# Two chained feed-forward layers after a short convolution: 64-row contraction terms as alternating half-array matmuls

## The chip, the cores and the metric

One core of one Trainium2 chip. The metric is the time of one execution on the device in microseconds; the kernel before takes 1338.2 us (median of 3 runs, 1337.74 to 1338.87).

## What is computed

`x` is 2 x 4096 rows of 192; `weight_gen` gives each row 8 heads with 7 taps. Cut to what matters:

```python
w = softmax(weight_gen)                                # over the 7 taps
x1 = einsum('bshk,bskhg->bshg', w, x_unf)              # causal 7-tap convolution, per head
h = np.maximum(x1 @ w_in, 0.0)                         # 192 -> 2048
x2 = h * h @ w_out                                     # 2048 -> 192
h = x2 @ w_in2
out = (h * np.cos(h)) @ w_out2
```

All in float32. On TensorE the kernel keeps the precision by splitting each operand into a rounded part (`_hi`) and the rest (`_lo`) and adding the products hi x hi, hi x lo and lo x hi.

## The kernel before

The 8192 tokens are 16 tiles of 512 (`TOK`). A layer's 2048 inner columns are 16 chunks of 128 (`SLOTS`), so each layer has 256 steps. Step n of layer 1 makes `h1` (one PSUM bank of two) from x1 (`up`, L363 to L370), squares its relu into `g1_hi` and `g1_lo`, and adds it into `y1` two slots later (`down`, L372 to L381). Layer 2 does the same with `h2`, `g2_*` and `y2`, 19 steps behind (`LAG`, L34), since its input x2 is the finished y1 of the tile. The program is a sequence of slots, written out per engine in a fixed order (`slot`, L399, L503, L648): slot i of tile t has step n = 16 t + i of layer 1 and m = n - 19 of layer 2. On TensorE a slot is up 1, down 1, up 2, down 2. The loop runs tiles 2 to 13; tiles 0 and 1 are written out because weights are still loaded and split, and the last four for the tail.

A row has 192 inputs: `DA` = 128 and `DD` = 64. An up is three matmuls over the 128 (L366 to L368), and two for the 64. For these `wd` holds the rounded weights in partitions 0 to 63 and their rest in 64 to 127, and the 64 inputs stand in both halves, so that L369 and L370 are full 128-row matmuls. To fill both halves the weights are loaded twice (L245, L246), x1's last 64 columns are written twice (L328, L643, turned by `turn_x1`), and x2's last 64 are copied to SBUF as `x2_d` and split for both halves (L532, L533 on ScalarE, L688 twice on VectorE), in slot `Y1_AT` + 1. Every matmul has 512 moving columns and its own 128 x 128 weights. A down is five: three into bank 0 of y for output columns 0 to 127, and two into bank 1, whose halves hold two partial sums of the last 64.

What orders the work is a semaphore per result. up 1 of step n waits for `g1_ready` of step n - 2 (its bank is then free), down 1 for `g1_ready` of its own step (L421), up 2 and down 2 likewise with `g2_ready` (L431, L447). up 2 of a new tile (slot `C2` = 3) waits for `x2_split` (L433). After y2 of a tile is done, slot `Y2_AT` = 5 copies it (L516, L661), and slots 6 and 7 transpose it on TensorE through a bank of h2 (`turn_out`, L396), which waits for the g2_lo of the step that used the bank (L441). Slots `TURN` = 13 and 14 transpose the next x1 (L386).

ScalarE and VectorE go through a slot in this order. ScalarE: sin of step m-1 (L510), y2 copy, relu (L521), x2 parts, x1_hi, g2_hi of m-1 (L542), g1_hi (L547), turns (rounding to whole turns, L552), output. VectorE: product with the cosine for m-1 (L655), y2 copy, relu square (L664), x2 and x1 parts, g2_lo of m-1 (L678), g1_lo (L683), x2's last 64 (L688), fraction of a turn (L693), output (L699). GpSimd convolves the next tile (L319, L325) and splits layer 2's weights.

Of the kernel before, what the change touches and what calls it, by code (L numbers as in the profile page):

```python
# [7 lines left out]
def conv_ffn_ffn_kernel(nc, x_d, gen_d, w_in1_d, w_out1_d, w_in2_d, w_out2_d, out_d):  # L8
# [29 lines left out]
    Y2_AT = C2 + D2  # L38
# [10 lines left out]
    INV_2PI = 1.0 / (2.0 * math.pi)  # L49
    assert DD * 2 == P and LAG % 2 == 1 and Y1_AT < C2  # L50
# [23 lines left out]
    with ctx:  # L74
# [12 lines left out]
        wd = [sb(f"wd{l}", [P, FF], F32R) for l in range(2)]  # L87
# [16 lines left out]
        x1 = sb("x1", [P, JJ, 2 * P])  # L104
# [3 lines left out]
        x1_hi = sb("x1_hi", [P, 2, 2, TOK], F32R)  # L108
        x1_lo = sb("x1_lo", [P, 2, 2, TOK], F32R)
        x2_hi = sb("x2_hi", [P, 2, 2, TOK], F32R)  # L110
        x2_lo = sb("x2_lo", [P, 2, 2, TOK], F32R)
# [10 lines left out]
        x2_d = sb("x2_d", [DD, TOK])[:, :]  # L122
# [12 lines left out]
        halo_zeroed = sem("halo_zeroed")  # L135
        ident_ready = sem("ident_ready")
# [39 lines left out]
        x2_d_ready = sem("x2_d_ready")  # L176
# [36 lines left out]

        def piece_lo(eng, pc, op):
# [4 lines left out]
            fs = slice(q * PF, (q + 1) * PF)  # L219
            eng.wait_ge(piece_hi[pc], op + 1)  # L220
            if op:
                eng.wait_ge(piece_ready[pc], op)
            if op == 0:
                last = eng.tensor_tensor(wa_lo[l][:, cols], stage_a[:, r, :], wa_hi[l][:, cols], ALU.subtract)
            elif op == 1:
                last = eng.tensor_tensor(wd[l][DD:P, cols], stage_d[DD:P, r, :], wd[l][DD:P, cols],
                                         ALU.subtract)
# [9 lines left out]
        def _(sp):  # L237
            def load_piece(pc):
# [6 lines left out]
                sp.dma_start(stage_d[0:DD, r, :], w_in_d[l][DA:DM, cols]).then_inc(piece_loaded[r], 16)  # L245
                sp.dma_start(stage_d[DD:P, r, :], w_in_d[l][DA:DM, cols]).then_inc(piece_loaded[r], 16)  # L246
# [30 lines left out]
            sp.wait_ge(first_sum, TAPS)  # L277
# [20 lines left out]
        def _(pool):  # L298
# [5 lines left out]
            STEP = 2 * TAPS - 1  # L304

            def convolve(t):
# [3 lines left out]
                products = [tap[:, k, :].rearrange("p (j d) -> p j d", d=DM) for k in range(2)]  # L310
                total = x1[:, :, 0:DM]
# [3 lines left out]
                for k in range(TAPS):  # L315
# [8 lines left out]
                    if k < TAPS - 1:  # L324
                        pool.tensor_tensor(total, products[0] if k == 1 else total, products[k % 2],  # L325
                                           ALU.add).then_inc(pool_step, 1)

                pool.tensor_tensor(x1[:, :, DM:2 * P], x1[:, :, DA:DM], products[(TAPS - 1) % 2][:, :, DA:DM],  # L328
                                   ALU.add).then_inc(pool_step, 1)
                pool.wait_ge(pool_step, STEP * (t - 1) + STEP)  # L330
                pool.tensor_tensor(total, total, products[(TAPS - 1) % 2], ALU.add).then_inc(x1_ready, 1)
# [30 lines left out]
        def _(pe):  # L362
            def up(o, l, f, hi, lo, par):  # L363

                f = slice(f * P, (f + 1) * P)
                pe.matmul(o, wa_hi[l][:, f], hi[:, par, 0, :], start=True, stop=False)  # L366
                pe.matmul(o, wa_hi[l][:, f], lo[:, par, 0, :], start=False, stop=False)  # L367
                pe.matmul(o, wa_lo[l][:, f], hi[:, par, 0, :], start=False, stop=False)  # L368
                pe.matmul(o, wd[l][:, f], hi[:, par, 1, :], start=False, stop=False)  # L369
                return pe.matmul(o, wd[l][:, f], lo[:, par, 1, :], start=False, stop=True)  # L370

            def down(y, l, f, hi, lo):  # L372
# [3 lines left out]
                part_a, part_d = y[:, 0, :], y[:, 1, :]  # L376
                pe.matmul(part_a, w[:, f, 0:DA], hi, start=first, stop=False)  # L377
                pe.matmul(part_a, w[:, f, 0:DA], lo, start=False, stop=False)  # L378
                pe.matmul(part_a, w[:, f, 2 * P:2 * DM], hi, start=False, stop=final)  # L379
                pe.matmul(part_d, w[:, f, DA:2 * P], hi, start=first, stop=False)  # L380
                return pe.matmul(part_d, w[:, f, DA:2 * P], lo, start=False, stop=final)  # L381

            def turn_x1(bank, part):

                for jj in range(JJ):
                    last = pe.transpose(h1[:, bank, jj * P:(jj + 1) * P], x1[:, jj, part * P:(part + 1) * P],  # L386
                                        ident[:, :])
# [11 lines left out]
            def slot(t, i, par):  # L399
                n = SLOTS * t + i  # L400
                m = n - LAG
                of = 1 - par if i >= C2 else par

                if live(n):
# [8 lines left out]
                    up(h1[:, i % 2, :], 0, i, x1_hi, x1_lo, par).then_inc(up1_done, 1)  # L413

                if TURN <= i < TURN + 2 and tile_live(t + 1) and live(n):
                    pe.wait_ge(x1_ready, t + 1)
                    pe.wait_ge(g1_ready, n)
                    turn_x1((i + 1) % 2, i - TURN).then_inc(x1_turned, 1)

                if live(n - D1):  # L420
                    pe.wait_ge(g1_ready, n - D1 + 1)  # L421
                    if i == D1 and counted(t):
                        pe.wait_ge(y1_read, t)
                    if isinstance(n, int) and n - D1 < SLOTS and (n - D1) % PF == 0:
                        pe.wait_ge(piece_ready[(n - D1) // PF], 3)
                    down(y1, 0, (i - D1) % SLOTS, g1_hi[:, (i - D1) % 2, :],
                         g1_lo[:, (i - D1) % 2, :]).then_inc(down1_done, 1)

                if live(m):
# [8 lines left out]
                    up(h2[:, (i - C2) % 2, :], 1, (i - C2) % SLOTS, x2_hi, x2_lo, of).then_inc(up2_done, 1)  # L438

                if OUT_AT <= i < OUT_AT + 2 and tile_live(t - 2):  # L440
# [19 lines left out]
            pe.wait_ge(first_sum, TAPS)  # L460
# [17 lines left out]
        def _(act):  # L478
            def piece_his(pc):
# [4 lines left out]
                act.wait_ge(piece_loaded[r], 64 * (pc // RING + 1))  # L484
                if l == 1:
                    act.activation(stage_a[:, r, :], stage_a[:, r, :], ACT.Copy,
                                   scale=INV_2PI).then_inc(piece_scaled, 1)
                    act.activation(stage_d[:, r, :], stage_d[:, r, :], ACT.Copy,
# [5 lines left out]
                act.activation(wd[l][:, cols], stage_d[:, r, :], ACT.Copy).then_inc(piece_hi[pc], 1)  # L494
# [8 lines left out]
            def slot(t, i, par):  # L503
# [4 lines left out]
                if live(m - 1):  # L508
                    act.wait_ge(fraction_ready, m)
                    act.activation(wave[:, 1 - c, :], wave[:, 1 - c, :], ACT.Sin,  # L510
                                   scale=2.0 * math.pi).then_inc(cos_ready, 1)
                if i == Y2_AT and tile_live(t - 2):
# [252 lines left out]
```

## Time and profile before

| | before |
|---|---|
| median of 3 runs | 1338.2 us |
| the profiled execution | 1338.88 us |
| its span, first to last instruction | 1337.1 us |
| mean granted TensorE clock | 0.987 |
| TensorE matmuls | 1257.4 us busy, 94% |
| VectorE | 991.4 us, 74% |
| ScalarE | 841.3 us, 63% |
| GpSimd | 379.1 us, 28% |

The profile is of one execution. Times are from the span's start; a line number is that of the kernel before. PE is TensorE's matmuls, PEld its weight loads, DVE VectorE, ACT ScalarE, POOL GpSimd. A recorded matmul is longer than the distance to the next one, since matmuls are pipelined and their ends are modelled: the distance of two starts is what counts. "Idle before" is the time an engine stood still before an instruction, and the releaser is what it had waited for.

### The profile page before, as it was taken

What the parts mean: (1) busy time and instruction counts of PE and PEld (TensorE: products, weight loads), DVE (VectorE), ACT (ScalarE), POOL (GpSimd) and SP (SyncE); (2) the same over time, 40 slices, a digit from 0 to 9 for tenths busy, and PEclk for the clock granted to TensorE, in tenths of its full rate; (3) what the DMA queues carried; (4) which work ended last, traced back from release to release, by engine and by line L of the source; (5) the groups of instructions that cost most, each with busy time, mean ns of one, the idle gap of its engine ahead of it and who ended that gap; (6) DMA issues with size and microseconds to landing.
All of it is one profiled execution on the core that took longest, in us unless ns stands there. A gap on an engine that the chain in (4) does not pass through costs nothing.

```text
span 1337.1 us, 17547 instructions
## 1 busy us (share of the span) xinstructions
PE 1257.4 (94%) x5392; PEld 993.1 (74%) x5392; DVE 991.4 (74%) x1487; ACT 841.3 (63%) x1535; POOL 379.1 (28%) x259
## 2 busy tenths in 40 slices
PE   3779999999999999999999999999999999999986
PEld 2557878778787877878787787878778787877754
DVE  7977777777777777777777777777777777777764
ACT  2487666666666666666666666666666666666654
POOL 3748530606023060502406051240605124000000
PEclk9889999999999999999999999999999999999998
DMA  5230000000100000010000001000000100000000
GB/s 163 79 122 1 30 30 13 30 13 0 41 0 29 12 30 12 0 41 0 30 12 29 12 0 41 0 29 12 30 12 0 41 0 1 13 1 13 1 12 12
DMA packets 14459, 31.80 MB, mean 24 GB/s; under 512 B 1605, under 2 KB 10051, under 8 KB 14273
## 3 DMA queue, kind: packets, MB, share of 16 engines
q1 hardware_dynamic: 14400, 31.19, 7.1%
q14 instruction: 43, 0.34, 0.1%
q8 instruction: 16, 0.26, 0.1%
HBM read 24.89 MB, written 6.29 MB: 23 GB/s over the span
## 4 chain that ended last, share of the span: by engine, by line
PE 60%; DVE 22%; ACT 10%; issue 6%; DMA 1%; ACTq 0%; DVEq 0%; SPq 0%
PE y L380 6%; PE y L378 6%; PE y L377 6%; PE y L381 6%; PE y L379 6%; PE h L366 6%; PE h L368 6%; PE h L370 6%; PE h L369 6%; PE h L367 6%; DVE turns L693 4%; DVE g_lo L678 4%; ACT turns L510 4%; ACT g_hi L542 3%; DVE h L655 3%
## 5 line engine op out<-in xcount | busy, mean ns | idle before, releaser
L319 POOL TENSOR_TENSOR tap<-xc,gen 128x768 f32<-128x768 f32 x105 | 162.0, 1549 | 689.0 <-PE h L386 666.3
L510 ACT ACTIVATE turns<-turns 128x512 f32<-128x512 f32 x256 | 161.9, 632 | 239.1 <-DVE turns L693 228.8
L655 DVE TENSOR_TENSOR h<-h,turns 128x512 f32<-128x512 f32 x256 | 179.2, 700 | 177.1 <-ACT turns L510 177.1
L366 PE MATMUL h<-x_hi,wa_hi 128*128 128x512 f32 x512 | 208.6, 407 | 39.2 <-DVE x_lo L688 18.9
L664 DVE SCALAR_TENSOR_TENSOR h<-h,relu 128x512 f32<-128x512 f32 x256 | 178.1, 696 | 63.9 <-ACT relu L521 63.9
L377 PE MATMUL y<-g_hi,wo 128*128 128x512 f32 x512 | 209.7, 410 | 7.1 <-DVE x_lo L670 3.2
L693 DVE SCALAR_TENSOR_TENSOR turns<-h,turns 128x512 f32<-128x512 f32 x256 | 176.2, 688 | 42.6 <-ACT turns L552 41.9
L368 PE MATMUL h<-x_hi,wa_lo 128*128 128x512 f32 x512 | 204.2, 399 | 0.0
L380 PE MATMUL y<-g_hi,wo 128*128 128x512 f32 x512 | 203.9, 398 | 0.0
L370 PE MATMUL h<-x_lo,wd 128*128 128x512 f32 x512 | 203.8, 398 | 0.0
L367 PE MATMUL h<-x_lo,wa_hi 128*128 128x512 f32 x512 | 203.7, 398 | 0.0
L378 PE MATMUL y<-g_lo,wo 128*128 128x512 f32 x512 | 203.4, 397 | 0.0
L369 PE MATMUL h<-x_hi,wd 128*128 128x512 f32 x512 | 203.2, 397 | 0.0
L381 PE MATMUL y<-g_lo,wo 128*128 128x512 f32 x512 | 203.1, 397 | 0.0
L379 PE MATMUL y<-g_hi,wo 128*128 128x512 f32 x512 | 203.0, 396 | 0.0
L521 ACT ACTIVATE relu<-h 128x512 f32<-128x512 f32 x256 | 151.6, 592 | 81.1 <-PE h L370 81.1
L678 DVE TENSOR_TENSOR g_lo<-h,g_hi 128x512 fp32r<-128x512 f32 x256 | 175.2, 684 | 30.0 <-ACT g_hi L542 25.9
L552 ACT ACTIVATE turns<-h 128x512 int32<-128x512 f32 x256 | 153.0, 598 | 69.0 <-PE h L370 66.9
L683 DVE TENSOR_TENSOR g_lo<-h,g_hi 128x512 fp32r<-128x512 f32 x256 | 175.9, 687 | 9.0 <-ACT g_hi L547 3.2
L547 ACT ACTIVATE g_hi<-relu 128x512 fp32r<-128x512 f32 x256 | 161.7, 632 | 28.7 <-PE y L381 11.7
L542 ACT ACTIVATE g_hi<-h 128x512 fp32r<-128x512 f32 x256 | 152.8, 597 | 28.6 <-DVE h L655 28.3
L366 PEld LDWEIGHTS h<-x_hi,wa_hi 128*128 128x128 f32 x512 | 97.0, 189 | 79.5 <-issue 26.4
(75 smaller groups left out, 1456.1 us busy)
## 6 DMA issues: line engine op xcount, KB each, us to landing
xc<-in_x_dram SPq DMA_DIRECT2D x14, 960.0 KB
out_dram<-arena SPq DMA_DIRECT2D x16, 384.0 KB, 2.3
arena<-in_moe_w_out_dram SPq DMA_DIRECT2D x16, 192.0 KB, 2.7
arena<-in_moe_w_in_dram SPq DMA_DIRECT2D x16, 128.0 KB, 2.4
arena<-in_moe_w_in_dram SPq DMA_DIRECT2D x32, 64.0 KB, 2.4
gen<-in_weight_gen_dram SPq DMA_DIRECT2D x1, 1568.0 KB, 10.6
xc<-in_x_dram SPq DMA_DIRECT2D x1, 768.0 KB
xc<-in_x_dram SPq DMA_DIRECT2D x2, 283.5 KB
```

What stands on the lines that cost most here:

```text
L366: pe.matmul(o, wa_hi[l][:, f], hi[:, par, 0, :], start=True, stop=False)
L367: pe.matmul(o, wa_hi[l][:, f], lo[:, par, 0, :], start=False, stop=False)
L368: pe.matmul(o, wa_lo[l][:, f], hi[:, par, 0, :], start=False, stop=False)
L369: pe.matmul(o, wd[l][:, f], hi[:, par, 1, :], start=False, stop=False)
L370: return pe.matmul(o, wd[l][:, f], lo[:, par, 1, :], start=False, stop=True)
L377: pe.matmul(part_a, w[:, f, 0:DA], hi, start=first, stop=False)
L378: pe.matmul(part_a, w[:, f, 0:DA], lo, start=False, stop=False)
L379: pe.matmul(part_a, w[:, f, 2 * P:2 * DM], hi, start=False, stop=final)
L380: pe.matmul(part_d, w[:, f, DA:2 * P], hi, start=first, stop=False)
L381: return pe.matmul(part_d, w[:, f, DA:2 * P], lo, start=False, stop=final)
L678: dve.tensor_tensor(g2_lo[:, 1 - c, :], h2[:, 1 - c, :], g2_hi[:, 1 - c, :], ALU.subtract).then_inc(g2_ready, 1)
L693: dve.scalar_tensor_tensor(wave[:, c, :], h2[:, c, :], 0.25, turns[:, c, :], ALU.add, ALU.subtract).then_inc(fraction_ready, 1)
```

## The change

- The d weights are held once: `wd_hi` and `wd_lo`, layer 1 in partitions 0 to 63, layer 2 in 64 to 127. `stage_d`, its scaling and its splits work on 64 partitions, and a piece is three DMAs instead of four.
- The inputs' last 64 rows stand likewise, in `xd_hi` and `xd_lo`, layer 1's in the lower half and layer 2's in the upper.
- An up is three 128-row matmuls (`up_a`) and three 64-row matmuls (`up_d`: hi x hi, lo x hi, hi x lo), which replace two 128-row ones. The six `up_d` of a slot alternate between layer 1, into a bank of h1, and layer 2, into a bank of h2.
- A slot on TensorE is up_a 1, up_a 2, six up_d, the x1 transposes if any, down 1, the output transposes if any, down 2. In the slots of `LATE` (2 and 4) down 2 comes ahead of down 1. down does its bank 1 first. down 1 of slot 2 waits for `x2_split` too.
- The copy of y2 moves from slot 5 to 4, the output transposes from 6 and 7 to 5 and 6.
- x2: in slot 1, ScalarE copies y1's other partial sum to `y1_part`, VectorE adds it in PSUM, and both parts of x2 are split from PSUM. The two copies and two subtractions on `x2_d` are gone.
- ScalarE's order in a slot is relu, turns, x1_hi, g1_hi, x2 parts, y2 copy, output, sin, d part of x2, g2_hi, the last of the same step m. VectorE's is g2_lo of m-1, relu square, fraction, x1_lo, g1_lo, x2 parts, y2 copy, output, product with the cosine.
- x1 has no doubled last 64 columns: one sum less on GpSimd per tile and on VectorE ahead of the first transposes; a padding of 64 columns is zeroed once.

```diff
--- before.py
+++ after.py
-    Y2_AT = C2 + D2
+    Y2_AT = C2 + D2 - 1
+    LATE = (Y1_AT + 1, Y2_AT)
...
-        wd = [sb(f"wd{l}", [P, FF], F32R) for l in range(2)]
+        wd_hi = sb("wd_hi", [P, FF], F32R)
+        wd_lo = sb("wd_lo", [P, FF], F32R)
...
-                sp.dma_start(stage_d[0:DD, r, :], w_in_d[l][DA:DM, cols]).then_inc(piece_loaded[r], 16)
-                sp.dma_start(stage_d[DD:P, r, :], w_in_d[l][DA:DM, cols]).then_inc(piece_loaded[r], 16)
+                sp.dma_start(stage_d[l * DD:(l + 1) * DD, r, :], w_in_d[l][DA:DM, cols]).then_inc(piece_loaded[r], 16)
...
-            def up(o, l, f, hi, lo, par):
+            def up_a(o, l, f, par):
 
                 f = slice(f * P, (f + 1) * P)
-                pe.matmul(o, wa_hi[l][:, f], hi[:, par, 0, :], start=True, stop=False)
-                pe.matmul(o, wa_hi[l][:, f], lo[:, par, 0, :], start=False, stop=False)
-                pe.matmul(o, wa_lo[l][:, f], hi[:, par, 0, :], start=False, stop=False)
-                pe.matmul(o, wd[l][:, f], hi[:, par, 1, :], start=False, stop=False)
-                return pe.matmul(o, wd[l][:, f], lo[:, par, 1, :], start=False, stop=True)
+                pe.matmul(o, wa_hi[l][:, f], xa_hi[l][:, par, :], start=True, stop=False)
+                pe.matmul(o, wa_hi[l][:, f], xa_lo[l][:, par, :], start=False, stop=False)
+                pe.matmul(o, wa_lo[l][:, f], xa_hi[l][:, par, :], start=False, stop=False)
+
+            def up_d(o, l, f, w, x, par, last):
+
+                rows = slice(l * DD, (l + 1) * DD)
+                return pe.matmul(o, w[rows, f * P:(f + 1) * P], x[rows, par, :], start=False, stop=last)
...
+                pe.matmul(part_d, w[:, f, DA:2 * P], hi, start=first, stop=False)
+                pe.matmul(part_d, w[:, f, DA:2 * P], lo, start=False, stop=final)
                 pe.matmul(part_a, w[:, f, 0:DA], hi, start=first, stop=False)
                 pe.matmul(part_a, w[:, f, 0:DA], lo, start=False, stop=False)
-                pe.matmul(part_a, w[:, f, 2 * P:2 * DM], hi, start=False, stop=final)
-                pe.matmul(part_d, w[:, f, DA:2 * P], hi, start=first, stop=False)
-                return pe.matmul(part_d, w[:, f, DA:2 * P], lo, start=False, stop=final)
+                return pe.matmul(part_a, w[:, f, 2 * P:2 * DM], hi, start=False, stop=final)
...
-                    up(h1[:, i % 2, :], 0, i, x1_hi, x1_lo, par).then_inc(up1_done, 1)
...
+                    up_a(o1, 0, f1, par)
                 if live(m):
...
+                    up_a(o2, 1, f2, of)
+
+                for w, x in ((wd_hi, xd_hi), (wd_lo, xd_hi), (wd_hi, xd_lo)):
+                    last = w is wd_hi and x is xd_lo
+                    if live(n):
+                        done1 = up_d(o1, 0, f1, w, x, par, last)
+                    if live(m):
+                        done2 = up_d(o2, 1, f2, w, x, of, last)
+                if live(n):
+                    done1.then_inc(up1_done, 1)
+                if live(m):
+                    done2.then_inc(up2_done, 1)
+
+                if TURN <= i < TURN + 2 and tile_live(t + 1) and live(n):
+                    pe.wait_ge(x1_ready, t + 1)
+                    pe.wait_ge(g1_ready, n)
+                    turn_x1((i + 1) % 2, i - TURN).then_inc(x1_turned, 1)
+
+                def down1():
+                    pe.wait_ge(g1_ready, n - D1 + 1)
+                    if i == D1 and counted(t):
+                        pe.wait_ge(y1_read, t)
+                        pe.wait_ge(x2_split, t)
+                    if isinstance(n, int) and n - D1 < SLOTS and (n - D1) % PF == 0:
+                        pe.wait_ge(piece_ready[(n - D1) // PF], 3)
+                    down(y1, 0, (i - D1) % SLOTS, g1_hi[:, (i - D1) % 2, :],
+                         g1_lo[:, (i - D1) % 2, :]).then_inc(down1_done, 1)
+
+                def down2():
+                    pe.wait_ge(g2_ready, m - D2 + 1)
+                    if i == Y2_AT + 1 and counted(t - 1):
+                        pe.wait_ge(y2_a_ready, t - 1)
+                        pe.wait_ge(y2_d_ready, t - 1)
+                    if isinstance(m, int) and m - D2 < SLOTS and (m - D2) % PF == 0:
+                        pe.wait_ge(piece_ready[PL + (m - D2) // PF], 3)
+                    down(y2, 1, (i - C2 - D2) % SLOTS, g2_hi[:, (i - C2 - D2) % 2, :],
+                         g2_lo[:, (i - C2 - D2) % 2, :]).then_inc(down2_done, 1)
+
+                if i in LATE and live(m - D2):
+                    down2()
+                if live(n - D1):
+                    down1()
                 if OUT_AT <= i < OUT_AT + 2 and tile_live(t - 2):
                     pe.wait_ge(g2_ready, at_most(m))
                     pe.wait_ge(y2_a_ready, t - 1)
                     pe.wait_ge(y2_d_ready, t - 1)
                     turn_out((i - C2 + 1) % 2, i - OUT_AT).then_inc(out_turned, 1)
-
-                if live(m - D2):
-                    pe.wait_ge(g2_ready, m - D2 + 1)
-                    if i == Y2_AT and counted(t - 1):
-                        pe.wait_ge(y2_a_ready, t - 1)
-                        pe.wait_ge(y2_d_ready, t - 1)
-                    if isinstance(m, int) and m - D2 < SLOTS and (m - D2) % PF == 0:
-                        pe.wait_ge(piece_ready[PL + (m - D2) // PF], 3)
-                    down(y2, 1, (i - Y2_AT) % SLOTS, g2_hi[:, (i - Y2_AT) % 2, :],
-                         g2_lo[:, (i - Y2_AT) % 2, :]).then_inc(down2_done, 1)
+                if i not in LATE and live(m - D2):
+                    down2()
 
...
-                if i == Y1_AT + 1 and tile_live(t - 1):
-                    act.wait_ge(x2_d_ready, t)
-                    act.activation(x2_hi[0:DD, 1 - par, 1, :], x2_d, ACT.Copy)
-                    act.activation(x2_hi[DD:P, 1 - par, 1, :], x2_d, ACT.Copy).then_inc(x2_hi_ready, 1)
...
+                if i == Y1_AT and tile_live(t - 1):
+                    act.wait_ge(y1_summed, t)
+                    act.activation(xd_hi[DD:P, 1 - par, :], y1[DD:P, 1, :], ACT.Copy).then_inc(x2_hi_ready, 1)
...
+                if i == Y1_AT and tile_live(t - 1):
+                    dve.wait_ge(y1_part_ready, t)
+                    dve.tensor_tensor(y1[DD:P, 1, :], y1[DD:P, 1, :], y1_part, ALU.add).then_inc(y1_summed, 1)
+                    dve.wait_ge(x2_hi_ready, 2 * t - 1)
+                    dve.tensor_tensor(xa_lo[1][:, 1 - par, :], y1[:, 0, :], xa_hi[1][:, 1 - par, :],
+                                      ALU.subtract).then_inc(y1_read, 1)
+                    dve.wait_ge(x2_hi_ready, 2 * t)
+                    dve.tensor_tensor(xd_lo[DD:P, 1 - par, :], y1[DD:P, 1, :], xd_hi[DD:P, 1 - par, :],
+                                      ALU.subtract).then_inc(x2_split, 1)
...
-                if i == Y1_AT + 1 and tile_live(t - 1):
-                    dve.wait_ge(x2_hi_ready, 2 * t)
-                    for half in range(2):
-                        last = dve.tensor_tensor(x2_lo[half * DD:(half + 1) * DD, 1 - par, 1, :], x2_d,
-                                                 x2_hi[0:DD, 1 - par, 1, :], ALU.subtract)
-                    last.then_inc(x2_split, 1)
```

## Rows read from the trace of the kernel before

**Rows 1.** The page: busy shares, then the span in 40 slices, in tenths.
```profile
PE 1257.4 (94%) x5392; PEld 993.1 (74%) x5392; DVE 991.4 (74%) x1487; ACT 841.3 (63%) x1535; POOL 379.1 (28%) x259
...
PE   3779999999999999999999999999999999999986
...
DVE  7977777777777777777777777777777777777764
...
PEclk9889999999999999999999999999999999999998
```

**Rows 2.** Timeline (start us, us, instruction) of a steady slot, and TensorE's L370 over all.
```profile
707.20 0.40 PE L366 MATMUL h<-x_hi,wa_hi 128*128 128x512 f32 x1
707.20 0.19 PEld L367 LDWEIGHTS h<-x_lo,wa_hi 128*128 128x128 f32 x1
...
707.43 0.39 PE L367 MATMUL h<-x_lo,wa_hi 128*128 128x512 f32 x1
...
711.87 0.40 PE L366 MATMUL h<-x_hi,wa_hi 128*128 128x512 f32 x1
...
L370 PE MATMUL h<-x_lo,wd 128*128 128x512 f32 x512 | 203.8, 398 | 0.0
```

**Rows 3.** Timeline of TensorE: the first matmul of the tile before that.
```profile
633.57 0.40 PE L366 MATMUL h<-x_hi,wa_hi 128*128 128x512 f32 x1
```

**Rows 4.** Timeline around x1 transposes (matmuls, weight loads) and output transposes.
```profile
703.03 0.39 PE L370 MATMUL h<-x_lo,wd 128*128 128x512 f32 x1
703.26 0.60 PE L386 MATMUL h<-ident,x 128*128 128x128 f32 x4
703.62 0.48 PE L377 MATMUL y<-g_hi,wo 128*128 128x512 f32 x1
703.94 0.39 PE L378 MATMUL y<-g_lo,wo 128*128 128x512 f32 x1
...
703.59 0.19 PEld L377 LDWEIGHTS y<-g_hi,wo 128*128 128x128 f32 x1
703.70 0.19 PEld L378 LDWEIGHTS y<-g_lo,wo 128*128 128x128 f32 x1
...
745.26 0.66 PE L396 MATMUL h<-ident,arena 128*128 128x128 f32 x4 [0.17 <-DVE g_lo L678]
```

**Rows 5.** TensorE's waits from 200 to 1180 us; the timeline at one of them.
```profile
PE h L366 <- DVE x_lo L688: 14.5, 12, 1.2
...
726.97 2.47 DVE L688 TENSOR_TENSOR x_lo<-x_d,x_hi 64x512 fp32r<-64x512 f32 x2
...
729.59 0.47 PE L366 MATMUL h<-x_hi,wa_hi 128*128 128x512 f32 x1 [1.22 <-DVE x_lo L688]
```

**Rows 6.** Timeline after a long wait of TensorE, near the start.
```profile
52.75 0.51 PE L366 MATMUL h<-x_hi,wa_hi 128*128 128x512 f32 x1 [4.10 <-DVE g_lo L683]
53.09 0.39 PE L367 MATMUL h<-x_lo,wa_hi 128*128 128x512 f32 x1
```

**Rows 7.** Timeline of VectorE in the loop, then of both in the tail.
```profile
720.92 0.68 DVE L678 TENSOR_TENSOR g_lo<-h,g_hi 128x512 fp32r<-128x512 f32 x1
...
721.52 0.68 DVE L683 TENSOR_TENSOR g_lo<-h,g_hi 128x512 fp32r<-128x512 f32 x1
...
1296.73 0.70 DVE L655 TENSOR_TENSOR h<-h,turns 128x512 f32<-128x512 f32 x1 [0.70 <-ACT turns L510]
1297.47 0.60 ACT L542 ACTIVATE g_hi<-h 128x512 fp32r<-128x512 f32 x1 [0.77 <-DVE h L655]
1297.96 0.59 ACT L552 ACTIVATE turns<-h 128x512 int32<-128x512 f32 x1
...
1299.42 0.63 ACT L510 ACTIVATE turns<-turns 128x512 f32<-128x512 f32 x1 [0.87 <-DVE turns L693]
1300.09 0.70 DVE L655 TENSOR_TENSOR h<-h,turns 128x512 f32<-128x512 f32 x1 [0.70 <-ACT turns L510]
```

**Rows 8.** Start: busy us (x count) of PE, PEld, DVE, ACT, POOL.
```profile
60.00:80.00 20.00, 15.24 (x60) 10.76 (x59) 19.10 (x31) 13.18 (x30) 7.03 (x9) 0.94 0.39 124
```

More of the change, by code:

```diff
@@ L103, in conv_ffn_ffn_kernel @@
         tap = sb("tap", [P, 2, JJ * DM])
-        x1 = sb("x1", [P, JJ, 2 * P])
+        x1 = sb("x1", [P, JJ * DM + DD])
         ident = sb("ident", [P, P])
         sin_ahead = sb("sin_ahead", [P, 1])
[L108 to L111, printed above, removed]
+        xa_hi = [sb(f"xa_hi{l}", [P, 2, TOK], F32R) for l in range(2)]
+        xa_lo = [sb(f"xa_lo{l}", [P, 2, TOK], F32R) for l in range(2)]
+        xd_hi = sb("xd_hi", [P, 2, TOK], F32R)
+        xd_lo = sb("xd_lo", [P, 2, TOK], F32R)
         relu = sb("relu", [P, 2, TOK])
@@ L225, in piece_lo @@
             elif op == 1:
-                last = eng.tensor_tensor(wd[l][DD:P, cols], stage_d[DD:P, r, :], wd[l][DD:P, cols],
+                last = eng.tensor_tensor(wd_lo[rows, cols], stage_d[rows, r, :], wd_hi[rows, cols],
                                          ALU.subtract)
@@ L309, in convolve @@
                 weights = gen[:, bass.ds(t * JJ * GEN, JJ * GEN)].rearrange("p (r k) -> p r k", k=TAPS)
[L310 to L311 removed]
+                total = x1[:, 0:JJ * DM]
                 pool.wait_ge(x1_turned, 2 * t)
@@ L483, in piece_his @@
                 cols = slice(q * PIECE, (q + 1) * PIECE)
-                act.wait_ge(piece_loaded[r], 64 * (pc // RING + 1))
+                rows = slice(l * DD, (l + 1) * DD)
+                act.wait_ge(piece_loaded[r], 48 * (pc // RING + 1))
                 if l == 1:
@@ L553, in slot @@
                                    bias=0.25).then_inc(turns_ready, 1)
+                if TURN <= i < TURN + 2 and tile_live(t + 1) and live(n):
+                    part = i - TURN
+                    act.wait_ge(x1_turned, 2 * t + 3 + part)
+                    act.activation(x1_part(xa_hi, xd_hi, 1 - par, part), turned_x1(1 - b, part),
+                                   ACT.Copy).then_inc(x1_hi_ready, 1)
+                if live(n):
+                    act.wait_ge(relu_done, n + 1)
+                    if counted(n - D1 + 1):
+                        act.wait_ge(down1_done, n - D1 + 1)
+                    act.activation(g1_hi[:, b, :], relu[:, b, :], ACT.Square).then_inc(g1_hi_ready, 1)
+                if i == Y1_AT and tile_live(t - 1):
+                    act.wait_ge(down1_done, SLOTS * t)
+                    if counted(t - 1):
+                        act.wait_ge(y1_summed, t - 1)
+                    act.activation(y1_part, y1[0:DD, 1, :], ACT.Copy).then_inc(y1_part_ready, 1)
+                    if counted(t - 2):
+                        act.wait_ge(up2_done, SLOTS * (t - 2))
+                    act.activation(xa_hi[1][:, 1 - par, :], y1[:, 0, :], ACT.Copy).then_inc(x2_hi_ready, 1)
+                if i == Y2_AT and tile_live(t - 2):
+                    act.wait_ge(down2_done, SLOTS * (t - 1))
+                    if counted(t - 2):
+                        act.wait_ge(out_turned, 2 * (t - 2))
+                    act.activation(y2_sb[:, 0, :], y2[:, 0, :], ACT.Copy).then_inc(y2_a_ready, 1)
                 if OUT_AT <= i < OUT_AT + 2 and tile_live(t - 2):
@@ L653, in slot @@
                 if live(m - 1):
-                    dve.wait_ge(cos_ready, m)
-                    dve.tensor_tensor(h2[:, 1 - c, :], h2[:, 1 - c, :], wave[:, 1 - c, :],
-                                      ALU.mult).then_inc(g2_made, 1)
+                    dve.wait_ge(g2_hi_ready, m)
+                    dve.tensor_tensor(g2_lo[:, 1 - c, :], h2[:, 1 - c, :], g2_hi[:, 1 - c, :],
+                                      ALU.subtract).then_inc(g2_ready, 1)
+                if live(n):
+                    dve.wait_ge(relu_done, n + 1)
+                    dve.scalar_tensor_tensor(h1[:, b, :], h1[:, b, :], 0.0, relu[:, b, :], ALU.max,
+                                             ALU.mult).then_inc(square_ready, 1)
@@ new lines, in slot @@
+                if live(m):
+                    dve.wait_ge(turns_ready, m + 1)
+                    dve.scalar_tensor_tensor(wave[:, c, :], h2[:, c, :], 0.25, turns[:, c, :], ALU.add,
+                                             ALU.subtract).then_inc(fraction_ready, 1)
+                if TURN <= i < TURN + 2 and tile_live(t + 1) and live(n):
+                    part = i - TURN
+                    dve.wait_ge(x1_hi_ready, 2 * t + 3 + part)
+                    dve.tensor_tensor(x1_part(xa_lo, xd_lo, 1 - par, part), turned_x1(1 - b, part),
+                                      x1_part(xa_hi, xd_hi, 1 - par, part), ALU.subtract).then_inc(x1_split, 1)
```

143 lines of the change are left out of this document (47 added, 96 removed).

## The prediction

> **What bounds the kernel now.** I read the page's busy shares and slices first. TensorE is at 9 tenths or more from the fourth slice to the next to last, at full granted clock after the start, while VectorE, the next busiest, sits at 7 and ScalarE is busy for 63% [rows 1]. So in the loop the span is made of matmuls, and only what TensorE does or waits for can move it. The timeline then gives the unit. A 512-column matmul starts 0.233 us after the one before it (the first two of a slot [rows 2]), and a steady slot, which is 20 of them, repeats after 711.87 - 707.20 = 4.67 us: 20 x 0.2333 = 4.667, so there is no hole in it. The weights of matmul k+1 begin to load when matmul k begins (PEld at 707.20, beside PE at 707.20), so loads are hidden.
>
> A tile takes 711.87 - 633.57 = 78.30 us [rows 2, 3]. Sixteen slots of 4.667 are 74.67. Two slots have four x1 transposes and two have four output transposes. From the first transpose of a group to the next matmul but one it is 703.94 - 703.26 = 0.68 against 0.233 without them, so about 0.43 each, 1.7 in all [rows 4]. What is left, 78.30 - 74.67 - 1.7 = 1.9, are waits. The wait list of TensorE in the loop names the largest: the first matmul of up 2 waits for the x2 split of L688, 14.5 us in 12 waits [rows 5]. In the timeline the two 64-row subtractions of L688 start at 726.97, take 2.47 together, and the matmul after them stands 1.22 us late [rows 5]. With its unhidden weight load (below) that is 1.4. The remaining 0.5 is next to the output transposes, which wait for the g_lo of the slot before (0.17 at 745.26 [rows 4]) and lose their hidden weight load to it.
>
> **The change, part by part.**
>
> *The 64-row terms.* Before, each up is 5 full matmuls, so two ups are 10. After, each is 3 full and 3 of 64 rows; layer 1 uses partitions 0 to 63, layer 2 uses 64 to 127, and they alternate into different banks. A joint slot issues 6 + 6 + 10 = 22. If two neighbours of different halves stream side by side, six take the time of three: 19 x 0.2333 = 4.433, a gain of 0.233 per slot. Joint slots are those in which both layers run: 256 - 19 = 237. So a perfect pairing is worth 237 x 0.233 = 55 us.
>
> No row of before has a 64-row matmul or two running together, so what pairing costs has to be bounded.
> - Lag of the second half: nothing, or one weight load if its weights can load only once the first half streams. The load is read from the transposes: each has 128 columns and a load of its own, and they follow each other at 0.108 us (four with a first-to-next-matmul time of 0.36, and loads at 703.59 and 703.70 [rows 4]). Weight loads therefore run at one per 0.11 us. Two per pair are 0.22, just under the 0.233 of streaming, so loads don't bound a steady pair.
> - Going from 128-row to 64-row work and back, twice a slot. From below: nothing. The nearest row is the change from full matmuls to transposes and back, another kind of operation on the same array, and it shows no gap beyond the loads (0.23 before the first transpose, 0.11 + 0.233 after the last [rows 4]). From above: the array runs empty and the next weight load isn't hidden. A matmul's recorded mean of 0.398 [rows 2] less its 0.233 of streaming is a tail of 0.165, and after a real idle the second matmul follows 0.34 after the first instead of 0.233, so the load adds 0.11 (52.75 to 53.09 [rows 6]). That is up to 0.27 per crossing.
>
> I take a lag of 0.108, because before never starts a load ahead of the preceding matmul, and 0.054 for the two crossings together, half an exposed load, because the nearest row shows none. The slot is then 4.433 + 0.162 = 4.595, which is 0.071 less than before: 237 x 0.071 = -17 us. Ends: -55 (all hidden), and for lag and two exposed loads, 0.324, +0.091 per slot, +22.
>
> *Both ups, then both downs.* ScalarE and VectorE get both results at once, and their orders are rewritten so that relu, turns, g1_hi, sin and g2_hi of one slot follow each other. The chain that repeats is relu, square, fraction, sin, cosine product, g2_hi, next relu. From the rows: a ScalarE result takes 0.59 to 0.63, a VectorE one 0.68 to 0.70, a handover 0.03, and an engine issues its next ready instruction after 0.49 (ScalarE, 1297.47 to 1297.96) or 0.60 (VectorE, 720.92 to 721.52) [rows 7]. Counting from the end of the ups: relu to 0.59, square 0.62, fraction 1.22 to 1.91, sin 1.95 to 2.58, product 2.61 to 3.31, g2_hi 3.34, so the next relu could go at 3.83, g2_lo done at 4.65. 3.83 is under 4.6, so a plain slot has 0.7 spare. g1_hi now waits for a down 1 that runs only after both ups; it ends some 1.3 after them, and the chain still closes in 3.83. In the two slots of LATE down 1 comes second and that is 1.2 later, the chain takes 4.9 to 5.5, and the slots behind absorb it.
>
> *x2 from PSUM.* The two copies and two slow subtractions on SBUF go (L688: 2.47 together); in their place one 64-row split read from PSUM, at the 0.68 of VectorE's other splits. In slot 1: y1 part, x2_hi, sum, x2_lo, d part: the last is ready some 4.6 us after slot 1's ups, and the first to need it is down 1 of slot 2, about 5.6 after them. up 2 of slot 3 comes later still. So the 1.4 us wait goes. Late next is the output: Y2_AT moves to 4, that slot also is in LATE, its g2_lo ends about 6.3 after its ups, and the transposes of slot 5 want it at 5.7. I put 0.65 of stall there in place of the 0.5 of now. Waits per tile go from 1.93 to 0.65; 1.28 x 14 loop tiles = -18 us.
>
> *Solo slots.* 19 at the start and 19 at the end run one layer, with nothing to pair: 11 matmuls instead of 10. At the end the slot is 3.36 us long (VectorE's L655 at 1296.73 and 1300.09), by the chain product, g2_hi, turns, fraction, sin [rows 7], which the change keeps; 2.57 plus crossings of matmuls still fit, so nothing. At the start VectorE is the full engine (19.1 of 20 us from 60 to 80, TensorE 15.2 [rows 8]); seven or so slots are matmul-bound, 0.233 plus crossings each: +3. The removed narrow add of VectorE ahead of the first transposes (L643), the d-piece DMA that is issued once instead of twice and GpSimd's removed add (it idles most of the loop, 28% busy [rows 1]) are within that rounding.
>
> Sum: 1338.9 (the profiled execution, span 1337.1) - 17 - 18 + 3 = 1306.9. The median of before is 0.7 lower, so 1306.
>
> **The rivals.**
>
> *The array runs empty at each crossing* (0.33 of my belief). Price: lag 0.108 and two tails of 0.165: 4.433 + 0.438 = 4.87, +0.20 x 237 = +48, with -18 + 3: 1372. With no lag 1346; with both loads exposed as well 1423. It decides from the point where lag and crossings exceed 0.233 + 15/237 = 0.30 us per slot. For it: no row shows a crossing of this sort, and two per slot make 474. Against it: the change to transposes and back costs nothing.
>
> The Trainium skill speaks for this rival: "TensorEngine Tiling (Array Packing)", section Key Properties, says that changing the tiling mode, not just the tile, drains the engine. No run here shows it yet; it gives no figure, and by the tail above the sum would be the 1372 of this rival instead of 1306. The same skill, "TensorE: Matmul & The Clock Gate", section on packing small matmuls, says that matmuls on different row groups run concurrently, which is what the 55 us need.
>
> *No side-by-side* (0.11). The six stream one after another: 22 x 0.2333 = 5.13, +0.467 x 237 = +111, so 1434, more with crossings. For it: every matmul in this trace starts a full stream after the last. Against it: all of these use all rows, so they had to.
>
> *The waits stay* (0.07). A shorter slot leaves ScalarE and VectorE less time to catch up after slots 1, 2 and 4, where I count chains up to 5.8 us, and stalls of today's size come back: 1306 + 18 = 1324.
>
> **How the numbers follow.** The forecast (0.49) has a range of its own of 1262 to 1328. At the low end everything of the pairs is hidden (-55) and nearly all waits go (-24, and +3 at the start). At the high end lag and one whole exposed load cost 0.216 a slot (-0.017 x 237 = -4) and half of the waits stay (-9, +3). Lag with both loads exposed (+22 - 18 + 3) is 1345 and meets the lower edge of the first rival. The range for all cases, 1262 to 1425, leaves out the serial case and the tips of the others, about 0.17. A measurement of this kernel can tell 0.2%, or 2.7 us, from no change. The seam between the forecast and the first rival gives 0.05 to no change, 0.02 from the one and 0.03 from the other. Faster is 0.47 + 0.07 = 0.54, slower 0.30 + 0.11 = 0.41.
>
> **What would show it.** Side by side is right if in the timeline six 64-row matmuls span 0.70 to 0.81 us and starts within a pair lie 0.0 to 0.11 apart; serial shows six starts at 0.233. The crossings are read from the last full matmul's start to the first 64-row start (0.23 if free, 0.40 if the array empties, 0.50 with the load), and the same at the way out. The L688 wait should have gone from the list and the wait of the output transposes grown to 0.65 per tile. A steady slot under 4.60 confirms the sum; 4.87 or 5.13 name the rivals. The forecast is wrong if the slot exceeds 4.73, or if ScalarE or VectorE hold TensorE in plain slots.

## The result: 1364.4 us, 2% slower

The changed kernel takes 1364.4 us (median of 4, 1363.7 to 1365.4) against 1338.0 beside it: a ratio of 1.0199, 95% interval 1.0181 to 1.0216. The forecast was 1306 and faster. The page of the changed kernel: spans, busy shares, then the slices that answer [rows 1].

```profile
span 1362.8 us, 18484 instructions
...
PE 1307.3 (96%) x5904; PEld 915.2 (67%) x5904; DVE 959.2 (70%) x1471; ACT 826.5 (61%) x1519; POOL 367.3 (27%) x244
...
PE   3888999999999999999999999999999999999997
...
PEclk9888999999999999999999999999999999999999
```

TensorE is busy for 50 us more, the engines beside it for less, and the clock is as before. The timeline of TensorE (start us, us, instruction) through one steady slot's 64-row part shows where, to be held against the 0.233 of [rows 2]:

```profile
724.55 0.40 PE L375 MATMUL h<-xa_hi,wa_lo 128*128 128x512 f32 x1
...
724.87 0.19 PEld L380 LDWEIGHTS h<-xd_hi,wd_hi 64*128 64x128 f32 x2 [0.37 <-issue]
724.88 0.51 PE L380 MATMUL h<-xd_hi,wd_hi 64*128 64x512 f32 x2
724.98 0.19 PEld L380 LDWEIGHTS h<-xd_hi,wd_lo 64*128 64x128 f32 x2
...
725.22 0.39 PE L380 MATMUL h<-xd_hi,wd_lo 64*128 64x512 f32 x2
...
725.45 0.40 PE L380 MATMUL h<-xd_lo,wd_hi 64*128 64x512 f32 x2
725.77 0.19 PEld L387 LDWEIGHTS y<-g_hi,wo 128*128 128x128 f32 x1 [0.36 <-issue]
725.77 0.50 PE L387 MATMUL y<-g_hi,wo 128*128 128x512 f32 x1
725.88 0.19 PEld L388 LDWEIGHTS y<-g_lo,wo 128*128 128x128 f32 x1
726.11 0.39 PE L388 MATMUL y<-g_lo,wo 128*128 128x512 f32 x1
...
729.68 0.50 PE L380 MATMUL h<-xd_hi,wd_hi 64*128 64x512 f32 x2
```

"x2" is a pair, merged because both start together. Pairs follow each other at 0.23 (725.22, 725.45): two 64-row matmuls for the price of one. But the way in costs 0.33 + 0.34 for two steps that would be 0.233 each (724.55, 724.88, 725.22), and the way out 0.32 + 0.34 (725.45, 725.77, 726.11). That is 0.19 to 0.20 per crossing, made of the same two parts each time. The first matmul of the new kind starts 0.09 late, and its weight load begins with it instead of under the matmul before. The second then comes 0.11 late, as after an idle [rows 6]. This slot is 729.68 - 724.88 = 4.80, and a plain slot of the loop takes 4.807 on average (19 x 0.2333 + 0.37) against 4.667.

Where the 25.7 us between the two spans come from, by the starts of the first up matmul of each slot (237 joint slots from slot 19 on):

| | before | after | difference |
|---|---|---|---|
| start up to the first joint slot | 102.4 | 109.0 | +6.6 |
| joint slots, at 4.667 and 4.807 | | | +33.2 |
| waits and transposes in them | | | -16.3 |
| tail | 77.7 | 79.9 | +2.2 |

The loop's tile goes from 78.3 to 79.4. TensorE's waits in the loop, to be held against the list in [rows 5], and slot 5 of one tile:

```profile
PE h L406 <- DVE g_lo L682: 7.6, 13, 0.7
...
755.64 0.39 PE L391 MATMUL y<-g_hi,wo 128*128 128x512 f32 x1
756.53 0.66 PE L406 MATMUL h<-ident,arena 128*128 128x128 f32 x4 [0.50 <-DVE g_lo L682]
```

The L688 wait is gone. What is late next is the g_lo of slot 4, for which the output transposes wait.

### The profile page after: what moved, and what is told of

Same layout as the page of the kernel before. It is cut to its first block, busy times and chain, and to the rows that moved or that the text cites. A ratio compares the mean times of both kernels' runs of the same rounds, so it can differ in the third digit from the quotient of the medians.

```text
span 1362.8 us, 18484 instructions
## 1 busy us (share of the span) xinstructions
PE 1307.3 (96%) x5904; PEld 915.2 (67%) x5904; DVE 959.2 (70%) x1471; ACT 826.5 (61%) x1519; POOL 367.3 (27%) x244
## 4 chain that ended last, share of the span: by engine, by line
PE 85%; DVE 8%; ACT 4%; issue 2%; DMA 1%; SPq 0%; DVEq 0%; ACTq 0%
PE h L380 16%; PE y L387 11%; PE y L391 8%; PE y L390 8%; PE y L389 8%; PE h L373 8%; PE y L388 8%; PE h L374 8%; PE h L375 8%; DVE g_lo L682 2%; DVE h L724 2%; PE h L397 1%; ACT g_hi L594 1%; PE h L406 1%; ACT g_hi L559 1%
## 5 line engine op out<-in xcount | busy, mean ns | idle before, releaser
L387 PE MATMUL y<-g_hi,wo 128*128 128x512 f32 x512 | 233.7, 456 | 6.9 <-DVE xd_lo L709 4.8
L373 PE MATMUL h<-xa_hi,wa_hi 128*128 128x512 f32 x512 | 206.9, 404 | 12.7 <-DVE g_lo L700 5.8
L374 PE MATMUL h<-xa_lo,wa_hi 128*128 128x512 f32 x512 | 204.3, 399 | 0.0
L391 PE MATMUL y<-g_hi,wo 128*128 128x512 f32 x512 | 203.7, 398 | 0.0
L375 PE MATMUL h<-xa_hi,wa_lo 128*128 128x512 f32 x512 | 202.9, 396 | 0.0
L389 PE MATMUL y<-g_hi,wo 128*128 128x512 f32 x512 | 202.8, 396 | 0.0
L387 PEld LDWEIGHTS y<-g_hi,wo 128*128 128x128 f32 x512 | 96.2, 188 | 106.0 <-issue 91.5
L380 PE MATMUL h<-xd_hi,wd_hi 64*128 64x512 f32 x512 | 139.5, 502 | 0.0
L373 PEld LDWEIGHTS h<-xa_hi,wa_hi 128*128 128x128 f32 x512 | 97.0, 189 | 47.4 <-DVE g_lo L682 9.5
```

Source lines behind the costliest of these rows:

```text
L373: pe.matmul(o, wa_hi[l][:, f], xa_hi[l][:, par, :], start=True, stop=False)
L374: pe.matmul(o, wa_hi[l][:, f], xa_lo[l][:, par, :], start=False, stop=False)
L375: pe.matmul(o, wa_lo[l][:, f], xa_hi[l][:, par, :], start=False, stop=False)
L380: return pe.matmul(o, w[rows, f * P:(f + 1) * P], x[rows, par, :], start=False, stop=last)
L391: return pe.matmul(part_a, w[:, f, 2 * P:2 * DM], hi, start=False, stop=final)
```

## The experiments

The theory after the result: a crossing between 128-row and 64-row work costs 0.20 us whatever is done between two of them, the pairs are really side by side, and the rest of the change is worth the 16 us in the joint slots. Its rivals: the new order of slots costs the time, or the 64-row matmuls themselves do.

### Full matmuls in place of the pairs

`up_full` is one matmul of `wa_lo` and `xa_lo` over 128 rows.

```diff
...
-                for w, x in ((wd_hi, xd_hi), (wd_lo, xd_hi), (wd_hi, xd_lo)):
-                    last = w is wd_hi and x is xd_lo
+                for k in range(2):
                     if live(n):
-                        done1 = up_d(o1, 0, f1, w, x, par, last)
+                        done1 = up_full(o1, 0, f1, par, k == 1)
                     if live(m):
-                        done2 = up_d(o2, 1, f2, w, x, of, last)
+                        done2 = up_full(o2, 1, f2, of, k == 1)
```

> The changed kernel with the six 64-row matmuls of a slot replaced by four 128-row ones on other operands (the products with the last 64 inputs are left out, a lo x lo product stands in their place): new order, old number of full streams, no crossing between 128 and 64 rows. Crossing theory: a steady slot is 20 x 0.2333 = 4.67 instead of 4.81, so 1364 - 35 in the joint slots and some 6 less in the solo slots at the start: 1323. Order theory (the new sequence on the engines costs the time): slots stay near 4.81 and the time near 1364.

Measured: 1328.0 us, ratio to before 0.9927 (0.9909 to 0.9944). Plain slots are 4.67, so the order of slots does not lengthen them. The start, up to the first joint slot, falls from 109.0 to 103.5 and the tail from 79.9 to 77.5, so most of their growth in the changed kernel comes from the 64-row work too. The sum missed by 5. About 2 of these are slot 5, which did not get shorter: it is 5.96 or 6.11 us here as in the changed kernel, so it isn't set by TensorE's work.

### Two pairs instead of three

```diff
-                for w, x in ((wd_hi, xd_hi), (wd_lo, xd_hi), (wd_hi, xd_lo)):
-                    last = w is wd_hi and x is xd_lo
+                for w, x in ((wd_hi, xd_hi), (wd_hi, xd_lo)):
+                    last = x is xd_lo
```

> The changed kernel with two pairs per slot instead of three (lo x hi of the last 64 left out). Crossing theory: a pair costs one stream, 0.233, and the crossings stay: slot 4.81 - 0.23 = 4.58, 1364 - 55 - 3 = 1306. If the extra time is spread over the pairs (0.13 each on top of the stream): slot 4.45, 1276.

Measured: 1315.7 us, ratio 0.9831 (0.9809 to 0.9852). The slot is 4.593, 0.21 less: a pair costs about one stream and the crossings stay. The sum missed by 10. The pair is 0.02 less than a full stream (4 us in all), slot 5 again stands at 5.96 to 6.12 (3 us), and slots 2 and 3, at 4.66 and 4.68, keep 2 us more.

### Four crossings instead of two

```diff
...
+            def up_c(o, l, f, par):
+
+                pe.matmul(o, wa_lo[l][:, f * P:(f + 1) * P], xa_hi[l][:, par, :], start=False, stop=False)
...
                     if live(m):
                         done2 = up_d(o2, 1, f2, w, x, of, last)
+                    if w is wd_hi and x is xd_hi:
+                        if live(n):
+                            up_c(o1, 0, f1, par)
+                        elif live(m):
+                            up_c(o2, 1, f2, of)
```

> The changed kernel with one full matmul of layer 1's up moved between the first pair and the second: same matmuls, four crossings per slot instead of two. Crossing theory: two more at 0.20 each, slot 4.81 + 0.40 = 5.21, +95 in the joint slots and up to 8 in the solo slots: 1459 to 1467. If what costs is entering 64-row work once per slot or the order of the engines: near 1364.

Measured: 1460.2 us, ratio 1.0915 (1.0868 to 1.0962), a slot of 5.22, 0.41 more for two crossings. One full matmul between two pairs, in the timeline:

```profile
731.58 0.40 PE L376 MATMUL h<-xa_hi,wa_lo 128*128 128x512 f32 x1
731.91 0.50 PE L385 MATMUL h<-xd_hi,wd_hi 64*128 64x512 f32 x2
732.34 0.50 PE L380 MATMUL h<-xa_hi,wa_lo 128*128 128x512 f32 x1
732.77 0.50 PE L385 MATMUL h<-xd_hi,wd_lo 64*128 64x512 f32 x2
733.11 0.39 PE L385 MATMUL h<-xd_lo,wd_hi 64*128 64x512 f32 x2
```

Steps of 0.43 where 0.233 was: each crossing adds its full 0.20. This is the run that fixes the price, as nothing but the place of one matmul differs.

### The same pairs, bunched in every other slot

```diff
...
-                for w, x in ((wd_hi, xd_hi), (wd_lo, xd_hi), (wd_hi, xd_lo)):
-                    last = w is wd_hi and x is xd_lo
+                terms = ((wd_hi, xd_hi), (wd_lo, xd_hi), (wd_hi, xd_lo)) * (2 if i % 2 == 0 else 0)
+                for k, (w, x) in enumerate(terms):
...
```

> The changed kernel with the same 64-row matmuls bunched: even slots issue six pairs, odd slots none (odd steps lack their last 64 inputs, even steps have them twice). Number of matmuls the same, crossings halved. Crossing theory (0.20 us each): 0.40 saved in every other slot, even slots 3.73 + 1.40 + 0.40 = 5.53, odd 3.73, so -0.40 x 118 = -47 in the loop, 1317, a little more if ScalarE and VectorE can't follow the short slots. If the 64-row matmuls themselves cost the time and not the crossings: no change, 1364.

Measured: 1342.7 us, ratio 1.0045 (1.0024 to 1.0065), half of the expected gain. The slots are as the theory has them: 5.53 and 3.73. But slot 5, an odd one, stays at 5.96 to 6.11 where 3.73 + 0.43 would do.

> The bunched kernel (six pairs in even slots, none in odd ones; odd steps lack their last 64 inputs) with the output transposes one slot later. Its even and odd slots were 5.53 and 3.73 as the crossing price of 0.20 says, but the total fell by 22 us, not 47. If the rest was slot 5's wait, 6.0 us against 3.73 + 0.43: 1343 - 26 = 1317. If bunching costs elsewhere: 1335 or more.

The edit, on top of the bunched kernel, is `OUT_AT = Y2_AT + 2`. Measured: 1321.3 us, ratio 0.9870 (0.9850 to 0.9890). Slots 5, 6 and 7 are now 3.73, 6.17 and 4.17. So the crossing price holds here too, and nearly all of the missing half was slot 5's wait. Even bunched, two slots take 9.26 against 9.33 with full matmuls.

### The output transposes one slot later

```diff
-    OUT_AT = Y2_AT + 1
+    OUT_AT = Y2_AT + 2
```

> The changed kernel with the output transposes one slot later (6 and 7 instead of 5 and 6), nothing else. If slot 5's length (5.96 to 6.11 us, with 64-row pairs, with full matmuls and with two pairs alike) is the wait for the g_lo of slot 4, it falls to 4.81, and slots 6 and 7 are 5.24: -0.8 x 14 = -11, 1353. If it is the copy of y2 or the first down 2 that holds it: no change.

Measured: 1353.5 us, ratio 1.0112 (1.0095 to 1.0129). Slot 5 is 4.81, slots 6 and 7 are 5.25, and TensorE's list of waits in the loop is empty. With all of TensorE's waits in the loop gone, the change is still 1.1% over before.

### Three of one half, then three of the other

```diff
-                for w, x in ((wd_hi, xd_hi), (wd_lo, xd_hi), (wd_hi, xd_lo)):
-                    last = w is wd_hi and x is xd_lo
+                terms = ((wd_hi, xd_hi), (wd_lo, xd_hi), (wd_hi, xd_lo))
+                for k, (w, x) in enumerate(terms):
                     if live(n):
-                        done1 = up_d(o1, 0, f1, w, x, par, last)
+                        done1 = up_d(o1, 0, f1, w, x, par, k == 2)
+                for k, (w, x) in enumerate(terms):
                     if live(m):
-                        done2 = up_d(o2, 1, f2, w, x, of, last)
+                        done2 = up_d(o2, 1, f2, w, x, of, k == 2)
```

> The changed kernel with the six 64-row matmuls in another order: three of layer 1 (partitions 0 to 63), then three of layer 2 (64 to 127). Same work, same number of crossings. If only matmuls of different halves that are neighbours stream side by side: the third and the fourth do, so five streams instead of three, +0.467 x 237 = +111, 1475. If the pairs were not side by side but merely recorded so, or if the array reordered them: 1364.

Measured: 1365.2 us, ratio 1.0205 (1.0161 to 1.0249), as the changed kernel. It is not the 1475 of a pairing between neighbours alone, but the 1364 of the other case. The timeline:

```profile
729.93 0.39 PE L375 MATMUL h<-xa_hi,wa_lo 128*128 128x512 f32 x1
730.25 0.51 PE L380 MATMUL h<-xd_hi,wd_hi 64*128 64x512 f32 x2
730.59 0.40 PE L380 MATMUL h<-xd_hi,wd_lo 64*128 64x512 f32 x2
730.82 0.40 PE L380 MATMUL h<-xd_lo,wd_hi 64*128 64x512 f32 x2
731.15 0.50 PE L387 MATMUL y<-g_hi,wo 128*128 128x512 f32 x1
```

The x2 of 730.25 are both `xd_hi, wd_hi`: the first and the fourth matmul of the program. The fourth starts with the first, 0.34 before the second. The third and the sixth, which are told apart by the semaphores that they raise, start at 730.82 and 730.83. So it is not that alternating order makes the pairs; matmuls of the idle half are started ahead of earlier ones of the busy half. Two things say so: the records, and the time, which would be 1475 otherwise. That the pairs were only recorded as side by side is excluded by the two-pair kernel, in which one pair less saves one stream and not two.

### x2 from PSUM alone, in the old order

```diff
...
+                        pe.wait_ge(x2_split, t)
...
-                if i == Y1_AT + 1 and tile_live(t - 1):
-                    act.wait_ge(x2_d_ready, t)
-                    act.activation(x2_hi[0:DD, 1 - par, 1, :], x2_d, ACT.Copy)
-                    act.activation(x2_hi[DD:P, 1 - par, 1, :], x2_d, ACT.Copy).then_inc(x2_hi_ready, 1)
...
+                if i == Y1_AT and tile_live(t - 1):
+                    act.wait_ge(x2_d_ready, t)
+                    act.activation(x2_hi[0:DD, 1 - par, 1, :], y1[DD:P, 1, :], ACT.Copy)
+                    act.activation(x2_hi[DD:P, 1 - par, 1, :], y1[DD:P, 1, :], ACT.Copy).then_inc(x2_hi_ready, 1)
...
-                    dve.tensor_tensor(x2_d, y1[0:DD, 1, :], x2_d, ALU.add).then_inc(x2_d_ready, 1)
+                    dve.tensor_tensor(y1[DD:P, 1, :], y1[DD:P, 1, :], x2_d, ALU.add).then_inc(x2_d_ready, 1)
```

VectorE's two subtractions likewise read y1 in PSUM and stand at the end of slot 1.

> The kernel before with one part of the change alone: the last 64 of x2 are summed in PSUM in slot 1 and split from there (two copies, two subtractions), down 1 of slot 2 waits for the split. Everything else, order and 128-row matmuls, as before. If the waits saved are a part of its own (14 x 1.2 to 1.4 us in the loop): 1338 - 18 = 1320, slot 3 down from 6.1 to 4.67 us, and no wait of the first up 2 matmul in the list. If the saving of the changed kernel came only with its new order of slots: 1338 as before.

Measured: 1349.1 us, ratio 1.0081 (1.0063 to 1.0099): slower than before, which neither side had. The list of waits, then the timeline at one and what follows it, then the windows (length, busy us (x count) of PE, PEld, DVE, ACT, POOL, granted clock, DMA):

```profile
PE y L377 <- DVE x_lo L693: 25.0, 12, 2.1
...
648.58 1.40 DVE L693 TENSOR_TENSOR x_lo<-y,x_hi 64x512 fp32r<-64x512 f32 x2
...
650.13 0.47 PE L377 MATMUL y<-g_hi,wo 128*128 128x512 f32 x1 [2.13 <-DVE x_lo L693]
...
651.65 0.63 PE L367 MATMUL h<-x_lo,wa_hi 128*128 128x512 f32 x1
652.08 0.63 PE L368 MATMUL h<-x_hi,wa_lo 128*128 128x512 f32 x1
...
651.40:655.00 3.60, 3.60 (x10) 2.79 (x9) 2.05 (x3) 1.28 (x3) 2.12 (x2) 0.53 0.13 21
655.00:660.00 5.00, 5.00 (x23) 4.03 (x22) 3.11 (x5) 2.90 (x5) 0.00 (x0) 1.00 0.49 183
```

The L688 wait has only moved. As long as the split reads PSUM, down 1 of the next tile may not overwrite y1, and in the old order it is wanted two microseconds too early. The subtractions themselves are fast now (1.40 for two, against the 2.47 of [rows 5]). A tile takes 78.7 against 78.3: slot 2 is 2.3 longer, and slots 3, 5 and 6 are 1.9 shorter. In two of the fourteen tiles the wait had a second price, which I trace under the last heading.

### The same with down 1 last in slot 2

> The first experiment (old order, x2 split from PSUM) with one more edit: in slot 2 down 1, which overwrites y1, goes behind up 2 and down 2. If the 2 to 4 us wait of that experiment in slot 2 is down 1 being too early for a split that still reads PSUM, it goes, since the split is ready about 2.1 us after down 1 was first wanted and the swap gives it 2.3: slots 2 and 3 at 4.67, 1320. If the split from PSUM is slow by itself, the wait stays: 1345 or more.

The edit, on top of the one above:

```diff
+                def down1():
...
+                if i != D1 and live(n - D1):
+                    down1()
...
+                if i == D1 and live(n - D1):
+                    down1()
```

`down1` holds the lines of down 1 as they were. The first call stands where down 1 was, the second behind down 2. Measured: 1312.2 us (4 runs, 1312.2 to 1313.1), ratio 0.9804 (0.9787 to 0.9820). It computes all of the reference, and is 2% under before and 3.8% under the changed kernel. A tile in the timeline, from its first matmul to the next one's:

```profile
622.01 0.40 PE L366 MATMUL h<-x_hi,wa_hi 128*128 128x512 f32 x1
...
698.45 0.40 PE L366 MATMUL h<-x_hi,wa_hi 128*128 128x512 f32 x1
```

76.44 us is 74.67 + 1.7 for the transposes: nothing is left but matmuls. The waits at the output transposes are gone too. The kernel of the experiment before had none either (slots 4 to 7 at 4.67, 4.67, 5.11, 5.10). I infer, without a run of its own, that the stall in slot 3 had made slots 5 and 6 late.

### Everything but the 64-row matmuls

The operands and the 128-row matmuls of before, with the changed kernel's order on all engines, x2 split from PSUM and the output transposes one slot later:

```diff
...
-                    up_a(o1, 0, f1, par)
+                    done1 = up_a(o1, 0, f1, par)
...
+                    for half in range(2):
+                        rows = slice(half * DD, (half + 1) * DD)
+                        last = dve.tensor_tensor(x2_lo[rows, 1 - par, 1, :], y1[DD:P, 1, :],
+                                                 x2_hi[rows, 1 - par, 1, :], ALU.subtract)
...
```

> All of the change except the 64-row matmuls, computed in full: the operands and five 128-row matmuls of an up as before, the new order of all engines, x2 split from PSUM, and the output transposes one slot later. No crossings and no waits: the loop's tile is 74.67 + 1.7 = 76.4 instead of 78.33, 1338 - 27 = 1311, and 1 more for the start. If the new order carries a cost of its own on TensorE: 1328 or more, as in the experiment with full rows.

Measured: 1330.6 us, ratio 0.9936 (0.9919 to 0.9953), 19 over the expectation, and where the rival case had put it (1328 or more). Steady slots are 4.67, so the new order doesn't slow TensorE's matmuls, but it has a price in a wait: slot 2 is 5.5 to 5.9. Its only wait in TensorE's list:

```profile
PE y L379 <- DVE x_lo L699: 8.8, 12, 1.0
```

With both halves to be filled again, slot 1 has one more copy and one more subtraction ahead of `x2_split`, and down 1 waits for it. That accounts for most of the 14.7 us that the joint slots take more than in the kernel with down 1 last (a tile takes 77.5 on average against 76.4). The rest is ahead of the first joint slot (1.9) and in the tail (2.7), and I have not followed it further. With the same matmuls, the new order is 18 us slower than the old one with down 1 last in slot 2.

## Why the prediction was wrong, point by point

- *What bounds the kernel.* Right: every difference found is in matmul streams, crossings and TensorE's waits.
- *Side by side, 55 us.* Right, and the 22 x 0.2333 rival fell: two pairs instead of three save 0.21 per slot, about one stream.
- *Lag of the second half, 0.108.* Wrong: none. The pair's loads start together (x2 at 724.87) and so do its matmuls, 0.003 apart in the records. I had taken the 0.108 between transposes for the distance that any two loads must keep; two halves load at once.
- *The crossings, 0.054 for both.* This is the step that failed. They cost 0.37 in the slot (0.41 for two in the four-crossings run). Lag and crossings together were put at 0.162, so the slot is 0.21 longer than forecast (4.807 against 4.595), x 237 = +50 us, and that alone turns -17 into +33. My bounds (0 to 0.27 per crossing) held the 0.20. The choice within them did not: I took the transposes for the nearest row, and they change the operation but not the rows in use. The fact that they showed no gap said nothing on this. The exposed load, for which I did have a row [rows 6], applies in full at every crossing, and the late start is 0.09, not the 0.165 of the recorded tail. That 0.165 was a reading of recorded ends, which are modelled and not measured.
- *The first rival* was the case that came, at 1364 against its 1372. That the numbers lie so close is in part luck. The 1372 is made of a lag of 0.108, which is not there, and two tails of 0.165, which measure 0.09, and it leaves out the two exposed loads of 0.11, which are there; the errors nearly cancel. Its break-even of 0.30 us per slot holds: with 0.37 the kernel is slower. The Trainium skill states in "TensorEngine Tiling (Array Packing)", Key Properties, that a change of the tiling mode drains the engine. The trace agrees that each change costs time, 0.20 each in the run with four crossings, but no run shows what the engine does in the 0.09 before the new load begins.
- *The waits, -18.* Right: waits and transposes are 16.3 less in the joint slots. The L688 wait went, and 0.78 per tile at the output transposes (a tile of 79.38 against 78.60 with these later) is left of 1.93, against the 0.65 forecast. The later transposes (1364.4 to 1353.5) show that it is the wait for slot 4's g_lo.
- *Solo slots, +3.* Too low: +6.6 at the start and +2.2 in the tail. A solo slot at the start is 2.95 instead of 2.33, a stream and two crossings; I had priced crossings there at the same 0.05. There nothing is paired, so the price is that of the change of rows and not of the pairing.
- *The chain of ScalarE and VectorE* has room in plain slots, as counted. The bunched kernel's plain short slots, at 3.73 for 16 streams, show that they follow even a single slot of that length between two of 5.53.

Faster had 0.54. The trace of before had no row for the one term that decided, and a range that held 0 to 0.27 for it should have given the two signs about even chances; the point was set near the wrong end.

## What to carry to other kernels

A split of the array into halves pays only for what runs between two changes of it. Going in and out costs 0.40 here, two crossings of 0.20. Three pairs in place of four full streams save one stream, 0.233, and lose; six pairs in place of eight, in one bunch per two slots, save 0.467 and come out 0.07 ahead (9.26 against 9.33). Ask of the nearest row whether it changes the same thing as the edit does.

When a result is read from PSUM to shorten a chain, name the next writer of that bank: the wait moves there. Here swapping one pair of downs in one slot of sixteen, with no change of the arithmetic, was worth 37 us (1349 to 1312).

## What was not expected of the hardware

- Matmuls of the two row halves were started out of program order: with three of one half and then three of the other, the fourth starts with the first (730.25), and the kernel is as fast as with alternation (1365.2 and 1364.4).
- A 64-row pair loads its weights together, with starts 0.003 apart, and each crossing costs 0.19 to 0.20 in either direction: 0.09 of a late start and 0.11 of an exposed load.
- In the x2 experiment, TensorE stood for 2.13 us at 650.13, and from 651.4 the granted clock had fallen to its lower level of 1.2 GHz: starts 0.43 apart (651.65, 652.08), mean granted clock 0.53 from 651.4 to 655. Slot 2 of that tile was 8.6 us instead of 7.0: the wait cost 1.6 more behind it. This came in only two of the fourteen tiles, at 177 and at 651. In the other twelve TensorE stood as long in slot 2 (6.95 to 7.03 us) and the clock stayed at its upper level, so the length of the wait alone does not decide it, and what does is open. It is worth 3 us of that kernel's time. Before, with waits of 1.2 us in the loop, and in the changed kernel the clock stayed at the upper level there.
